# Attention and two feed-forward stages on one core: normalising ahead of the next maximum, and the q copy on ScalarE

## The chip, the cores and the metric

One core of a Trainium2 chip. The time is the device time of the whole kernel in microseconds; of a kernel's runs the median counts.

## What is computed

Windowed and pooled attention over q, k, v of shape (2, 8, 576, 64), then a routed mixture of 8 experts, then a feed-forward layer. The change lies in the attention, of which this is the core:

```python
factor = 4
q_d = q.reshape(B, H, Sd, factor, D).mean(axis=3)        # k_d, v_d alike
out_d = sm_attn(q_d, k_d, v_d)                           # softmax attention, pooled
out_up = np.repeat(out_d, factor, axis=2)
mask = np.abs(pos[:, None] - pos[None, :]) < factor
scores = scale * np.matmul(q, k.transpose(0, 1, 3, 2))   # scale = 1/8
scores = np.where(mask, scores, -1000000000.0)
scores = scores - np.max(scores, axis=-1, keepdims=True)
attn = np.exp(scores)
attn = attn / (np.sum(attn, axis=-1, keepdims=True) + 1e-09)
out_local = np.matmul(attn, v)
return (out_up + out_local).astype(np.float32)
```

Its result, as 1152 tokens of 512 numbers, is routed to one expert each (`w1`, ReLU, `w2`, times the gate), and the outcome goes through `x @ w_in`, `h * tanh(softplus(h))`, `@ w_out`.

## The kernel before

Each engine has its own program, a block of instructions in a fixed order, and they meet at semaphores. The attention handles the 1152 tokens in 9 tiles of 128. Its work is cut into 15 steps, written out in the list `STEPS`: 9 local steps (one tile each, all 8 heads, a window of 70 keys for each 64 queries) and 6 pooled steps ("down") in the order local 0 to 3, three down, three down, local 4 to 8. A loop `for n in range(ROUNDS)`, with 19 rounds, runs on every engine and spreads each step over several rounds.

TensorE in round n: some warming matmuls on constant data (`keep_warm`, rounds 0 to 9), `scores(n)`, the transposes of k and then q of tile n + 2 (rounds 0 to 6, `transpose_k`, L1116; `transpose_q`, L1108), from round 9 on the transposes and logits for the router, `attend` of an earlier step, and `probs_t(n - 1)`, the transposes of the probabilities (L1173 for a local step, L1168 for a pooled one). `probs_t` of a local step waits for `s_nrm`, that is for `norm` of its step on VectorE; that of a pooled step waits for the exponentials alone, as its factor is applied later, in `od_copy`. It also waits for `s_ptc`, the copy of the transposed probabilities before it. `scores(n)` waits for the exponentials of step n - 2 and for the copies of q and k; round 4 and round 7, the first pooled steps of each batch, also for the pooled sums (`s_qd`). In rounds 10 to 14 the counts of the router stand in the middle of `scores(n)` and wait for VectorE's one-hot sums (`s_cum`, L938).

VectorE in round n: `stats(n)` (the negated row maximum of the scores, from PSUM, L881 or L877 and L879; in rounds 10 to 14 behind `read_counts`), `q_copy(n + 2)` (q times 1/8 from PSUM into `qT`, L854), `norm(n - 1)` (L888, sum plus a small number; L890, its reciprocal; L893, in local steps, probabilities times the reciprocal), the router's `place`, `pooled` sums of q and k over 4 tokens (L840; tile 0 in round 0, tile 1 in round 1, tiles 2 and 3 in round 2, tile 4 in round 3, and so on to tiles 7 and 8 in round 6), `od_copy` and `route`.

ScalarE in round n: the router's copies and exponential, `k_copy(n + 2)` (L646), `exps(n)` (8 exponentials of 70 columns or 4 of 144, L663, each with its row sum), `pt_copy(n - 1)` (the transposed probabilities out of PSUM, L646) and `x_copy` (the attention's output, L646). `exps(n)` waits for the maximum of its step (`s_mx`).

GpSimd builds constant rows, adds up v for the pooled steps (`sum_v`, L545 to L548), places pooled outputs and scatters rows of x to the experts. SyncE's queue issues the loads in a fixed order: q and k of tiles 0 to 5, v for the pooled steps, tiles 6 to 8 (from tile 3 on a load waits until the tile three before it has been transposed), more v, the router's weights, 22 loads of windows of v (L422), zeros for the experts' rows, and then the experts' weights.

Of the kernel before, what the change touches and what calls it, by code (L numbers as in the profile page):

```python
# [7 lines left out]
P = 128  # L8
# [6 lines left out]
ALU = mybir.AluOpType  # L15
# [118 lines left out]
def build(nc, q, k, v, w_gate, w1, w2, w_in, w_out, consts, consts16, out, cap):  # L134
# [12 lines left out]
    with ctx:  # L147
# [134 lines left out]
        def turned(n):  # L282

            return n + 2 if 0 <= n < NT - 2 else None
# [356 lines left out]
        def _(act):  # L641
# [3 lines left out]
            def copy(dst, src):  # L645
                return nc.scalar.activation(dst, src, ACT.Copy)  # L646

            def k_copy(t):
                act.wait_ge(s_tk, t + 1)
                copy(kT[:, :, HALO + t * P:HALO + (t + 1) * P],  # L650
                     ps[:, qk_banks(t)[1], :].rearrange("p (h t) -> p h t", h=HP)).then_inc(s_kTc, 1)
# [47 lines left out]

            for t in range(2):  # L700
                k_copy(t)
            act.wait_ge(s_cb, 5)
            for n in range(ROUNDS):
                if x_turn(n) is not None:
                    xt_copy(x_turn(n))
                if count_turn(n) is not None and n < ROUNDS - 1:
                    gate_exp(count_turn(n))
                if turned(n) is not None:
                    k_copy(turned(n))
                if n < NS:  # L710
                    exps(n)
                if is_local(n - 2) and n - 2 in attended(n):
                    x_copy(n - 2)
                if 0 <= n - 1 < NS:
                    pt_copy(n - 1)
                for m in attended(n):
                    if is_local(m) and m != n - 2:
                        x_copy(m)
# [102 lines left out]
        def _(dve):  # L821
# [27 lines left out]
                    last = red(kdT[:, :, kcol:kcol + cnt], kT[:, :, HALO + lo:HALO + lo + n])  # L849
                last.then_inc(s_qd, 1)  # L850

            def q_copy(t):
                dve.wait_ge(s_tq, t + 1)
                V.tensor_scalar(qT[:, :, t * P:(t + 1) * P], ps[:, q_bank(t), :].rearrange("p (h t) -> p h t", h=HP),  # L854
                                SCALE, None, ALU.mult).then_inc(s_qTc, 1)

            def views(n):

                s0 = 2 * (n % 2)
# [105 lines left out]
                need(gate)  # L965
                V.tensor_scalar(x_sb[:, t, :], x_sb[:, t, :], r_gate[:, c], None, ALU.mult).then_inc(s_gx, 1)

            for t in range(2):
                q_copy(t)
            for n in range(ROUNDS):  # L970
                if n < NS:
                    stats(n, count_turn(n))
                if turned(n) is not None:
                    q_copy(turned(n))
                if 0 <= n - 1 < NS:
                    norm(n - 1)
                if count_turn(n) is not None:
                    if n >= NS:
                        read_counts(count_turn(n))
# [470 lines left out]
```

## Time and profile before

| | |
|---|---|
| median of 3 runs | 483.32 us (481.43 to 490.93) |
| profiled execution, as timed | 488.61 us |
| its span, first to last instruction | 486.5 us |
| mean granted clock of TensorE | 0.966 |
| TensorE matmul busy | 454.6 us, 93% of the span |
| VectorE busy | 275.3 us, 57% |
| ScalarE busy | 229.3 us, 47% |
| GpSimd busy | 134.9 us, 28% |

A row of the timeline gives a start and a duration in us from the span's start, the engine (PE is TensorE, DVE VectorE, ACT ScalarE, POOL GpSimd, SPq SyncE's queue), the line, the operation, and what it writes and reads; the last brackets are the idle time in front of it and who ended it. A granted clock of 1.00 is 2.4 GHz, 0.50 is 1.2 GHz. An instruction's duration has a fixed tail that overlaps with the next one's start, so that the distance between two starts is what one costs in a row of its like.

### The profile page before, as it was taken

Reading aid. Unit: us, or ns where it says so; the run is one execution under the profiler, and the core shown is the slowest. Engines: PE = TensorE matmul, PEld = TensorE weight load, DVE = VectorE, ACT = ScalarE, POOL = GpSimd, SP = SyncE. Lnnn points to the kernel's source line nnn. Section 1 sums busy time; section 2 is a strip of 40 time slices with the busy share of each in tenths; the row PEclk is TensorE's granted clock in tenths of the full one; section 3 lists DMA queues with packets and bytes.
Section 4 is the critical chain, followed back from the end, with each engine's and each line's share of the span. In section 5 each row is a group of like instructions: output and inputs, shape, how many; then the busy total and the mean of one; then the engine's idle time right before and its main releaser. Section 6 shows DMA issues by size and latency. Waiting matters only on the chain.

```text
span 486.5 us, 10257 instructions
## 1 busy us (share of the span) xinstructions
PE 454.6 (93%) x3520; PEld 420.3 (86%) x3521; DVE 275.3 (57%) x660; ACT 229.3 (47%) x629; POOL 134.9 (28%) x133
## 2 busy tenths in 40 slices
PE   9756899988879999999999999999999999999993
PEld 8645798778779999999999988899999888899982
DVE  5575647878211111011111399888888888888883
ACT  2653467860312333233224366665655565765541
POOL 8484332412000000000000565433352223443202
PEclk9876999997989999999999999999999999999998
DMA  9969898412558799897775314231232121141001
GB/s 186 190 117 170 156 369 287 154 66 101 194 173 293 265 348 328 276 328 268 269 243 188 121 44 83 48 87 44 88 108 86 43 80 50 54 142 43 1 0 65
DMA packets 72001, 74.87 MB, mean 154 GB/s; under 512 B 32800, under 2 KB 47776, under 8 KB 71968
## 3 DMA queue, kind: packets, MB, share of 16 engines
q1 hardware_dynamic: 70240, 69.71, 48.4%
q0 software_dynamic: 1728, 4.72, 2.5%
q8 instruction: 20, 0.33, 0.3%
q14 instruction: 13, 0.11, 0.1%
HBM read 64.98 MB, written 9.44 MB: 153 GB/s over the span
## 4 chain that ended last, share of the span: by engine, by line
PE 85%; DVE 8%; issue 2%; ACT 2%; DMA 1%; POOL 0%; POOLq 0%; SPq 0%; ACTq 0%; DVEq 0%
PE ps L1097 79%; PE ps L1173 1%; PE ps L1312 1%; DVE pr L893 1%; PE ps L1116 1%; PE ps L1168 1%; PE ps L1108 1%; DVE qT L854 1%; DMA xg<-x_by_expert 1%; DMA x_by_expert<-x_sb,xslot 1%; DVE sme L888 1%; PE ps L1218 0%; ACT pr L663 0%; ACT prT L646 0%; DVE kdT L840 0%
## 5 line engine op out<-in xcount | busy, mean ns | idle before, releaser
L597 POOL TENSOR_TENSOR wiL<-raw,wiH 128x512 fp32r<-128x512 f32 x48 | 62.4, 1302 | 259.5 <-ACT wiH L646 156.1
L1097 PE MATMUL ps<-hid,raw 128*128 128x128 f32 (+2 forms) x512 | 72.3, 301 | 3.4 <-issue 3.4
L1097 PEld LDWEIGHTS ps<-hid,raw 128*128 128x128 f32 x512 | 70.4, 195 | 3.6 <-issue 3.6
L1097 PE MATMUL ps<-xe,raw 128*128 128x128 f32 (+2 forms) x512 | 70.3, 298 | 1.4 <-issue 0.8
L1097 PEld LDWEIGHTS ps<-xe,raw 128*128 128x128 f32 x512 | 68.8, 191 | 2.3 <-issue 1.4
L1097 PE MATMUL ps<-x2L,wiH 128*128 128x384 f32 x192 | 65.3, 340 | 0.0
L1097 PE MATMUL ps<-x2H,wiH 128*128 128x384 f32 x192 | 65.1, 339 | 0.2 <-DVE x2L L1013 0.2
L1097 PE MATMUL ps<-x2H,wiL 128*128 128x384 f32 x192 | 64.6, 337 | 0.0
L1097 PE MATMUL ps<-woH,gH 128*128 (+1 forms) x144 | 56.9, 395 | 1.9 <-DVE gL L1013 1.9
L1097 PE MATMUL ps<-woH,gL 128*128 (+1 forms) x144 | 57.1, 397 | 0.0
L1097 PE MATMUL ps<-woL,gH 128*128 (+1 forms) x144 | 56.7, 394 | 0.0
L1013 DVE TENSOR_TENSOR woL<-wo_in,woH 128x1024 f32 x8 | 9.8, 1226 | 81.2 <-ACT woH L646 81.2
L785 ACT ACTIVATE md<-mg 128x384 f32<-128x384 f32 x48 | 25.3, 526 | 43.3 <-DVE mg L1068 43.2
L741 ACT ACTIVATE hid<-ps 128x128 f32<-128x128 f32 (+2 forms) x64 | 18.6, 301 | 51.5 <-PE ps L1097 47.2
L1050 DVE TENSOR_SCALAR mu<-ps 128x384 f32<-128x384 f32 x48 | 26.7, 557 | 25.3 <-PE ps L1097 25.3
L1097 PEld LDWEIGHTS ps<-x2H,wiH 128*128 128x128 f32 x192 | 36.0, 188 | 2.4 <-issue 0.5
L1013 DVE TENSOR_TENSOR x2L<-ps,x2H 128x128 f32 (+2 forms) x32 | 9.3, 321 | 50.8 <-ACT x2H L646 50.7
L1097 PEld LDWEIGHTS ps<-x2L,wiH 128*128 128x128 f32 x192 | 36.1, 188 | 1.9
L646 ACT ACTIVATE gH<-ps 128x384 fp32r<-128x384 f32 x48 | 23.6, 492 | 26.9 <-DVE ps L1074 26.9
L1097 PE MATMUL ps<-warmb 128*128 128x160 bf16 x320 | 33.1, 277 | 3.3 <-DVE kdT L840 1.8
L1097 PEld LDWEIGHTS ps<-x2H,wiL 128*128 128x128 f32 x192 | 36.0, 188 | 0.0
L1097 PEld LDWEIGHTS ps<-warmb 128*128 128x128 bf16 x320 | 30.8, 119 | 4.1 <-issue 3.0
(130 smaller groups left out, 770.7 us busy)
## 6 DMA issues: line engine op xcount, KB each, us to landing
raw<-in_moe_w SPq DMA_DIRECT2D x32, 1024.0 KB, 6.4
raw<-in_moe_w_in SPq DMA_DIRECT2D x24, 512.0 KB, 3.7
x_by_expert<-x_sb SPq DMA_DIRECT2D x1, 4608.0 KB, 15.8
xg<-x_by_expert SPq DMA_DIRECT2D x8, 512.0 KB, 3.7
wo_in<-in_moe_w_out SPq DMA_DIRECT2D x8, 512.0 KB, 7.4
v<-in_v SPq DMA_DIRECT2D x4, 576.0 KB
qk_tok<-in_k SPq DMA_DIRECT2D x8, 256.0 KB, 4.4
qk_tok<-in_q SPq DMA_DIRECT2D x8, 256.0 KB, 5.0
```

The costliest lines, as they stand in the source:

```text
L597: nc.gpsimd.tensor_tensor(wiL[:, r, :, :], raw_wi_tile(r), wiH[:, r, :, :].bitcast(F32), ALU.subtract).then_inc(s_wil, 1)
L646: return nc.scalar.activation(dst, src, ACT.Copy)
L741: nc.scalar.activation(hid[:, m, 0:w], ps[:, m % 4, 0:w], ACT.Relu).then_inc(s_hr, 1)
L785: nc.scalar.activation(d, mg[:, r1, :], ACT.Ln, bias=2.0).then_inc(s_ln, 1)
L854: V.tensor_scalar(qT[:, :, t * P:(t + 1) * P], ps[:, q_bank(t), :].rearrange("p (h t) -> p h t", h=HP), SCALE, None, ALU.mult).then_inc(s_ ...
L888: V.tensor_scalar(st(sme), st(sm), f, f * EPS, ALU.mult, ALU.add).then_inc(s_den, 1)
L893: V.tensor_tensor(pb, pb, st(rc).unsqueeze(3).to_broadcast(shape), ALU.mult).then_inc(s_nrm, 1)
L1013: V.tensor_tensor(dst, whole, high.bitcast(F32), ALU.subtract).then_inc(sem_, 1)
L1050: V.tensor_scalar(mu[:, r, :], ps[:, 3 + r, 0:SW], MISH_CAP, None, ALU.min).then_inc(s_uc, 1)
L1097: return T.matmul(out_, a, b, start=start, stop=stop, skip_group_check=True)
L1108: last = T.transpose(ps[:, q_bank(t), hp * P:(hp + 1) * P], qk_tok[:, slot3, 0, hp * P:(hp + 1) * P], ident)
L1116: last = T.transpose(ps[:, qk_banks(t)[1], hp * P:(hp + 1) * P], qk_tok[:, slot3, 1, hp * P:(hp + 1) * P], ident)
```

## The change

VectorE's `q_copy` goes to ScalarE, where it stands behind `k_copy` of the same tile and in front of `exps`, as an activation Copy with scale 1/8; the first two are made ahead of the loop, as before. On VectorE, `norm(n - 1)` moves to the head of the round, in front of `stats(n)`.

```diff
--- before.py
+++ after.py
@@ -645,6 +645,11 @@
             def copy(dst, src):
                 return nc.scalar.activation(dst, src, ACT.Copy)
 
+            def q_copy(t):
+                act.wait_ge(s_tq, t + 1)
+                nc.scalar.activation(qT[:, :, t * P:(t + 1) * P], ps[:, q_bank(t), :].rearrange("p (h t) -> p h t", h=HP),
+                                     ACT.Copy, scale=SCALE).then_inc(s_qTc, 1)
+
             def k_copy(t):
                 act.wait_ge(s_tk, t + 1)
                 copy(kT[:, :, HALO + t * P:HALO + (t + 1) * P],
@@ -699,6 +704,7 @@
 
             for t in range(2):
                 k_copy(t)
+                q_copy(t)
             act.wait_ge(s_cb, 5)
             for n in range(ROUNDS):
                 if x_turn(n) is not None:
@@ -707,6 +713,7 @@
                     gate_exp(count_turn(n))
                 if turned(n) is not None:
                     k_copy(turned(n))
+                    q_copy(turned(n))
                 if n < NS:
                     exps(n)
                 if is_local(n - 2) and n - 2 in attended(n):
@@ -849,11 +856,6 @@
                     last = red(kdT[:, :, kcol:kcol + cnt], kT[:, :, HALO + lo:HALO + lo + n])
                 last.then_inc(s_qd, 1)
 
-            def q_copy(t):
-                dve.wait_ge(s_tq, t + 1)
-                V.tensor_scalar(qT[:, :, t * P:(t + 1) * P], ps[:, q_bank(t), :].rearrange("p (h t) -> p h t", h=HP),
-                                SCALE, None, ALU.mult).then_inc(s_qTc, 1)
-
             def views(n):
 
                 s0 = 2 * (n % 2)
@@ -965,15 +967,11 @@
                 need(gate)
                 V.tensor_scalar(x_sb[:, t, :], x_sb[:, t, :], r_gate[:, c], None, ALU.mult).then_inc(s_gx, 1)
 
-            for t in range(2):
-                q_copy(t)
             for n in range(ROUNDS):
+                if 0 <= n - 1 < NS:
+                    norm(n - 1)
                 if n < NS:
                     stats(n, count_turn(n))
-                if turned(n) is not None:
-                    q_copy(turned(n))
-                if 0 <= n - 1 < NS:
-                    norm(n - 1)
                 if count_turn(n) is not None:
                     if n >= NS:
                         read_counts(count_turn(n))
```

## Rows read from the trace of the kernel before

**Rows 1.** The page's 40 slices of the span: TensorE's busy tenths, its granted clock.

```profile
PE   9756899988879999999999999999999999999993
...
PEclk9876999997989999999999999999999999999998
```

**Rows 2.** Windows by stage: busy us (instructions) of each engine, granted clock, DMA share, GB/s.

```profile
12.50:60.00 47.50, 34.17 (x361) 28.96 (x358) 30.14 (x56) 23.73 (x101) 23.96 (x26) 0.78 0.85 157
60.00:75.00 15.00, 15.00 (x263) 13.18 (x262) 6.21 (x22) 8.79 (x30) 6.87 (x13) 1.00 1.03 350
```

**Rows 3.** Waits of TensorE, 11 to 60 us: waited for, us in all, times, longest.

```profile
PE ps L1173 <- DVE pr L893: 11.1, 4, 3.7
```

**Rows 4.** Timeline of TensorE: start us, us, instruction, [idle before, ended by].

```profile
13.95 0.99 PE L1097 MATMUL ps<-warmb 128*128 128x160 bf16 x12 [0.41 <-ACT kT L646]
...
15.76 0.66 PE L1116 MATMUL ps<-cst,qk_tok 128*128 128x128 f32 x4
...
18.87 1.08 PE L1173 MATMUL ps<-cst,pr 128*70 128x128 f32 x8 [2.02 <-DVE pr L893]
19.75 1.80 PE L1097 MATMUL ps<-warmb 128*128 128x160 bf16 x12
...
27.54 1.92 PE L1173 MATMUL ps<-cst,pr 128*70 128x128 f32 x8 [3.34 <-DVE pr L893]
...
45.41 1.92 PE L1173 MATMUL ps<-cst,pr 128*70 128x128 f32 x8 [3.74 <-DVE pr L893]
...
51.49 0.82 PE L1168 MATMUL ps<-cst,pr 96*72 96x96 f32 x8
...
58.76 1.27 PE L1097 MATMUL ps<-warmb 128*128 128x160 bf16 x16 [1.66 <-DVE kdT L840]
...
105.24 1.04 PE L1173 MATMUL ps<-cst,pr 128*70 128x128 f32 x8
```

**Rows 5.** Timeline of VectorE, rounds 1, 2 and 4.

```profile
15.90 0.74 DVE L881 TENSOR_REDUCE mx<-ps 128x8 f32<-128x560 f32 x1 [0.44 <-PE ps L1097]
16.89 0.69 DVE L854 TENSOR_SCALAR qT<-ps 128x512 f32<-128x512 f32 x1 [0.25 <-PE ps L1108]
17.50 0.16 DVE L888 TENSOR_SCALAR sme<-sm 128x8 f32<-128x8 f32 x1
...
17.93 0.80 DVE L893 TENSOR_TENSOR pr<-pr,rc 128x560 f32<-128x560 f32 x1
...
24.84 0.85 DVE L888 TENSOR_SCALAR sme<-sm 128x8 f32<-128x8 f32 x1
...
25.96 1.52 DVE L893 TENSOR_TENSOR pr<-pr,rc 128x560 f32<-128x560 f32 x1
...
42.32 1.25 DVE L888 TENSOR_SCALAR sme<-sm 128x8 f32<-128x8 f32 x1
```

**Rows 6.** Timeline of ScalarE: the first and the last of round 1's exponentials.

```profile
16.95 0.31 ACT L663 ACTIVATE pr<-ps,mx 128x70 f32<-128x70 f32 x1
...
19.21 0.25 ACT L663 ACTIVATION_READ_ACCUMULATOR pr<-ps,mx 128x1 f32 x1
```

**Rows 7.** A window after the first stall, columns as in rows 2.

```profile
19.75:23.10 3.35, 3.35 (x49) 2.76 (x46) 0.17 (x1) 1.02 (x1) 0.57 (x2) 0.50 0.95 202
```

**Rows 8.** ScalarE's k copies as a group: busy us, mean ns, idle before.

```profile
L646 ACT ACTIVATE kT<-ps 128x512 f32<-128x512 f32 x9 | 5.4, 602 | 22.6 <-PE ps L1116 22.6
```

**Rows 9.** Timeline of GpSimd: copies, then the first and last of six sums.

```profile
15.28 5.04 POOL L564 COPY raw<-cst 32x512 f32<-32x512 f32 x8 [3.94 <-DMA cst<-in_consts]
24.40 1.26 POOL L545 TENSOR_TENSOR vd<-v 72x512 f32<-72x512 f32 x1 [4.08 <-DMA v<-in_v]
...
31.33 1.26 POOL L548 TENSOR_TENSOR vd<-vd,v4s 72x512 f32<-72x512 f32 x1
```

**Rows 10.** Waits of TensorE, 75 to 116 us, columns as in rows 3.

```profile
PE ps L1097 <- DVE cum L938: 2.6, 5, 0.8
```

**Rows 11.** Timeline of the queue of loads (SyncE): the windows of v.

```profile
37.45 22.27 SPq L422 DMA_DIRECT2D vwin<-in_v  x22
```

## Prediction

> **What bounds the kernel now.** I read the page's slices first [rows 1]: TensorE is busy in nine tenths or more of most slices, and the clock that it is granted is down to 0.6 to 0.8 in the second to fourth slice, that is from 12 to 49 us. The windows by stage say the same in microseconds [rows 2]: from 12.5 to 60 us TensorE works 34.17 of 47.5 us at a mean clock of 0.78, from 60 to 75 us 15.00 of 15.00 at 1.00. From the twelfth slice on nearly all is TensorE's own work, and the change doesn't touch it. So I look at the first 60 us, and a little at 75 to 116 us.
>
> Who ends TensorE's idle time there is in the waits [rows 3]: four times, 11.1 us in all, the transposes of the probabilities (L1173, `probs_t`) wait for the multiplication on VectorE (L893, in `norm`). One more wait, 1.66 us in front of 58.76 [rows 4], is for the pooled sums of k (L840). The timeline of TensorE [rows 4] gives the order of one round: warming matmuls and scores (from 13.95), transposes of k and q of the tile after next (15.76), then `probs_t` of the round before (18.87), 2.02 us late. VectorE's rows [rows 5] say why: it takes the maximum (15.90), then waits for the q transposes to copy q (16.89), and only then normalises (17.50 to 18.73). ScalarE [rows 6] is ready long before: the exponentials of round 1 run from 16.95 to 19.46 and are normalised at 24.84, in round 2. So the stall is an order on VectorE: `norm(n-1)`, ready long before, stands behind `stats(n)` and `q_copy(n+2)`, which need TensorE's newest work. `probs_t` of rounds 0 to 3 should come one TensorE round apart; it starts at 18.87 and, three rounds later, at 45.41 [rows 4], 8.85 us apart.
>
> Each of these stalls is followed by matmuls at the lower clock [rows 7]: 19.75 to 23.10 at 0.50 (1.2 GHz), after an idle 2.02 us. Twelve warming matmuls take 1.80 us there and 0.99 us at 13.95 at the higher level (2.4 GHz) [rows 4]; sixteen took 1.27 us at 58.76, so that after 1.66 us of idleness the clock was still the higher one.
>
> **The change part by part.**
>
> *q copy to ScalarE.* Nine copies leave VectorE, 0.69 us each [rows 5]; ScalarE copies k from the same kind of PSUM bank in 602 ns [rows 8], 0.5 us from start to start. I take 0.5 us of ScalarE for each q copy, between 0.5 (a k copy's pitch) and 0.69 (VectorE's time), 4.5 to 6.2 us in all. ScalarE sat idle 22.6 us in front of the k copies alone, so it has room; but the copy stands in front of `exps(n)`, so it delays them by 0.5 to 0.7 us where the maximum is there already. In the first two copies, ahead of the loop, 26 warming matmuls cover it: nothing.
>
> *norm ahead of the maximum.* The new chain goes in a circle: `exps(n)` 2.5 us (16.95 to 19.46 [rows 6]), `norm(n)` 1.23 us, `stats(n+1)` 0.75 us [rows 5], with hand-overs of 0.05 to 0.1 us: 4.6 us a round. TensorE's round at full clock is 1.81 for warming and scores (13.95 to 15.76), 0.93 for the transposes (0.49 and 0.44, the k transposes' pitch and the q's) and 0.88 for `probs_t` (18.87 to 19.75), 3.6 us [rows 4]; at the lower one 3.35 (19.75 to 23.10 [rows 7]) and, doubled, 1.7 and 1.7: 6.8 us. What waits behind `norm` on VectorE is the maximum, behind it ScalarE's exponentials, and behind these the copy of the transposed probabilities: nothing that TensorE needs in the same round.
>
> How long `norm` takes depends on GpSimd. At 17.50 to 18.73 it took 1.23 us; at 24.84 to 27.48 it took 2.64 us (the small L888 0.85 instead of 0.16, L893 1.52 instead of 0.80 [rows 5]), and GpSimd's first sums of v, six in a row, run from 24.40 to 32.6 [rows 9]. In round 4 the small one alone took 1.25 (42.32), about 3.0 in all. The same instructions in the same place would give both prices again, so I use 2.64 inside 24.4 to 32.6 us and 1.23 outside.
>
> The Trainium skill, "GPSIMD Engine Reference", section Key points, says that GpSimd shares its SBUF interfaces with VectorE and contends with instructions that have two SBUF inputs, which L893 is. By that rule alone the normalisation at 17.93, under GpSimd's copies (15.28 to 20.3 [rows 9]), would be slow too; the row has 0.80 us there, so only the sums are charged. Were every one of the four charged, the sum would be 2.8 us smaller.
>
> *The walk.* Round 0: the k copy ends just before 13.95, where TensorE was waiting for it; the q copy behind it lets `exps(0)` start at about 14.2 and end at 16.7. Round 1: `norm(0)` 16.75 to 18.0, `probs_t(0)` at 18.1 (was 18.87); maximum to 18.75, `exps(1)` 18.8 to 21.3. Round 2: TensorE's transposes end at 18.1 + 0.88 + 1.81 + 0.93, with their tail 21.9; `norm(1)` runs 21.3 to 22.65, before the sums of v begin; `probs_t(1)` at 22.75 (was 27.54). Maximum to 23.35, `exps(2)` to 25.9. Round 3: TensorE is through at 26.6, `norm(2)` is charged 2.64: `probs_t(2)` at 28.6, idle 2.0 us. Maximum to 29.25, pooled sums of tile 4 to 30.6, and the warming matmuls of round 4 start there. `exps(3)` to 31.8, `norm(3)` partly charged: `probs_t(3)` at 34.0 (was 45.41): 11.4 us early. Round 5 at full clock is 0.88 + 1.1 + 0.66 + 0.93 = 3.6 us, so `probs_t(4)` is at 37.7 (was 51.49); from there to the end of `probs_t(5)` it is 5.6 us (51.49 to 58.76 less 1.66 [rows 4]): 43.3. The 1.66 us wait for pooled sums behind it shrinks to about 0.3, since VectorE no longer has the q copy in front. Warming matmuls of round 7 at 43.6 instead of 58.76: 15.2 us.
>
> One stall of the walk, 2.0 us, is as long as the ones after which the clock fell. A fall would put some 4 us of TensorE's work at half speed, half of it inside waits: 2 us back. I take that: 13.2 us.
>
> *Rounds 7 to 11* have next to no idle TensorE (15.00 of 15.00 us from 60 to 75 [rows 2]) and don't change: `norm` first finds `exps` done and fills the time in which VectorE waits for the scores. *Rounds 12 to 14*: VectorE's one-hot sums hold the counts up for 2.6 us in five waits [rows 10]. `norm` now runs while VectorE waits for the scores, so the sums come earlier, until TensorE's own round is the limit. Three of the five waits lie where no scores are left and stay. Between 0 (the sums hang on the logits anyway) and 1.0 us (two, of 0.52 us on average); I take 0.9.
>
> *Moved transfers.* The queue of loads issues 22 loads of v in 22.27 us from 37.45 on [rows 11]; a load ahead of them waits for the transposes of tile 5, which the walk brings from about 34 (27.54 + 1.7 + 3.35 + 1.3) to 26.5. With the loads between, they start some 5 us earlier, at 32.5; eleven of them, one batch, are issued by 43.6, and the first use is in round 8, after 51 us. That covers the landing; nothing is charged. If they did not move at all, 2 to 3 us would be lost.
>
> Sum: 13.2 + 0.9 = 14.1 us from the profiled execution, 486.5 us of span and 488.61 us as timed: 474.5. The median before, 483.32, is 5.3 us below that execution. If none of this difference lies in the first 60 us, the median goes to 469.2. If part of it is a clock that fell less often, that part can't be won: a mean clock of 0.78 is 0.44 of 47.5 us at half speed, 21 us, of which up to 13 can be idle, so the clock cost between 4 and 10 us there. I discount 14.1 to 11.8 and predict 471.5 us.
>
> **The rivals.**
>
> *The clock stays low.* With every round at 6.8 us TensorE itself is the limit: `probs_t(3)` at 18.1 + 3 x 6.8 = 38.5, 6.9 us early, plus 1.3 and 0.9: 9.1 us from the profiled execution. Discounted like the forecast, 475.5 (473.5 to 479). For: the walk leaves stalls of 1.3 and 2.0 us. Against: 1.66 us did no harm. The same time comes out if the executions of the kernel before that make the median had a high clock: then its rounds take 3.6 + 0.7 (q copy) + 1.23 or 2.64 (`norm`) + 0.15, 5.7 to 7.1 us, against 4.6 to 5.9, so about 5 + 1.3 + 0.9 = 7 us in all. Together 0.25.
>
> *Transfers become the bound*: qk tiles or v blocks land late. The mean DMA share is 0.85 in 12.5 to 60 us [rows 2], and TensorE has no wait for a load among its waits. Against that, the shift asks for the same bytes sooner. 4 to 8 us back of the 11.8: 475.5 to 479.5. Chance 0.12.
>
> *The circle is the new bound and gives nothing.* From `probs_t(0)` to `probs_t(14)` the rounds average 6.2 us now (18.87 to 105.24 [rows 4]). If exponentials, normalisation and maximum take 6.2 us in each, nothing is won: about 483. That needs `norm` charged everywhere and slow hand-overs. Chance 0.08.
>
> *Slower.* The same circle in all 14 rounds at 6.9 us or more gives 0.7 x 14 = 10 us: 493. It decides where `norm` passes 3.5 us; the longest in rows 5 is about 3.0, in one round. Chance 0.04.
>
> **How the numbers follow.** Forecast 0.51, with its own range of 466 to 474.5. About 2% (9.7 us, below 473.7) is what a measurement can tell. Faster takes most of the forecast's share and some of the first two rivals': 0.57. Slower: 0.04. Same: 0.39. The range 466 to 479.5 leaves out the last two rivals and thin tails.
>
> **What would show it.** Right: the waits of TensorE for L893's successor fall from 11.1 us to under 5; `probs_t` of round 3 starts near 34; the granted clock between 20 and 50 us is above 0.9; the gap in front of round 7's warming matmuls is under 1 us; the expert phase starts 12 to 15 us earlier. Wrong: TensorE waits for the transposed probabilities' copy or for k and q to land; the clock in 20 to 50 us is still near 0.7; ScalarE's exponentials wait for the maximum for more than 1 us in rounds 7 to 14.

## The result and the profile after

| | before | after |
|---|---|---|
| median of the first comparison | 484.50 us (481.43 to 490.93, 4 executions) | 478.50 us (477.59 to 479.58, 4) |
| ratio after/before, 95% interval | | 0.9881, 0.9833 to 0.9929 |
| profiled execution, as timed | 488.61 us | 479.58 us |
| span | 486.5 us | 477.5 us |
| mean granted clock of TensorE | 0.966 | 0.982 |

The kernel became 1.2% faster. It was timed twice more, with the same sign: 476.64 us (ratio 0.9879) and 478.09 us (0.9832). The medians here are of all executions, while the ratios leave out slow ones, more than 1.5% above the fastest of the same kernel. The forecast was 471.5 us: the time lies in the range of 466 to 479.5 us, but the gain came out at half to four fifths of what was forecast. It was 6.0, 9.5 and 8.0 us by the medians of the three comparisons and about 6, 6 and 8 us by the ratios, instead of 11.8.

The slices of the span on the profile's page, TensorE's busy tenths and its granted clock, which answer [rows 1]:

```profile
PE   9778999878699999999999999999999999999993
...
PEclk9979899999999999999999999999999999999998
```

The windows by stage (columns as in [rows 2]), with a window of 5.2 us behind the longest stall:

```profile
12.50:60.00 47.50, 39.73 (x532) 34.79 (x522) 30.11 (x61) 32.12 (x127) 28.61 (x34) 0.89 0.98 166
60.00:75.00 15.00, 15.00 (x262) 13.37 (x261) 11.16 (x49) 10.09 (x44) 4.04 (x8) 1.00 1.04 377
...
31.30:36.50 5.20, 5.17 (x32) 4.61 (x33) 3.41 (x7) 2.60 (x10) 4.51 (x6) 0.50 1.00 207
```

TensorE is busy for 39.73 of the first 47.5 us instead of 34.17, at a clock of 0.89 instead of 0.78. Its waits from 11 to 60 us, against [rows 3]:

```profile
PE ps L1171 <- DVE pr L895: 4.5, 3, 2.5
PE ps L1095 <- DVE kdT L847: 2.8, 2, 1.8
```

The waits for the normalised probabilities fell from 11.1 to 4.5 us. The waits for the pooled sums of k grew from 1.8 us in all (0.16 and 1.66) to 2.8 us (0.98 and 1.84). TensorE's timeline, with the rows that answer [rows 4]:

```profile
18.61 1.04 PE L1171 MATMUL ps<-cst,pr 128*70 128x128 f32 x8 [1.45 <-DVE pr L895]
19.48 0.99 PE L1095 MATMUL ps<-warmb 128*128 128x160 bf16 x12
...
22.94 1.07 PE L1171 MATMUL ps<-cst,pr 128*70 128x128 f32 x8 [0.55 <-DVE pr L895]
...
29.28 1.07 PE L1171 MATMUL ps<-cst,pr 128*70 128x128 f32 x8 [2.53 <-DVE pr L895]
31.33 2.29 PE L1095 MATMUL ps<-warmb 128*128 128x160 bf16 x16 [0.98 <-DVE kdT L847]
...
36.52 1.49 PE L1171 MATMUL ps<-cst,pr 128*70 128x128 f32 x8
...
48.08 2.29 PE L1095 MATMUL ps<-warmb 128*128 128x160 bf16 x16 [1.84 <-DVE kdT L847]
```

`probs_t` of rounds 0 to 3 starts at 18.61, 22.94, 29.28 and 36.52 instead of 18.87, 27.54, 36.04 and 45.41. Sixteen warming matmuls take 2.29 us at 31.33 and at 48.08, against 1.27 us at 58.76 in [rows 4]: the clock fell twice, once behind idle times of 2.53 and 0.98 us with only `probs_t`, still at the higher clock, between them, and once behind 1.84 us. VectorE, against [rows 5] (the multiplication of rounds 0 and 1, then round 2):

```profile
17.61 0.85 DVE L895 TENSOR_TENSOR pr<-pr,rc 128x560 f32<-128x560 f32 x1
...
22.14 0.74 DVE L895 TENSOR_TENSOR pr<-pr,rc 128x560 f32<-128x560 f32 x1
...
26.12 1.19 DVE L890 TENSOR_SCALAR sme<-sm 128x8 f32<-128x8 f32 x1 [0.21 <-ACT pr L668]
...
27.59 1.64 DVE L895 TENSOR_TENSOR pr<-pr,rc 128x560 f32<-128x560 f32 x1
```

The normalisation of round 2 lies under GpSimd's sums and lasts from 26.12 to about 29.2, 3.1 us. ScalarE's copies as groups (against [rows 8]) and the loads of v (against [rows 11]):

```profile
L646 ACT ACTIVATE kT<-ps 128x512 f32<-128x512 f32 x9 | 5.5, 611 | 12.8 <-PE ps L1114 12.8
L650 ACT ACTIVATE qT<-ps 128x512 f32<-128x512 f32 x9 | 5.4, 605 | 0.3 <-PE ps L1106 0.3
```

```profile
34.86 22.68 SPq L422 DMA_DIRECT2D vwin<-in_v  x22
```

A q copy costs ScalarE 605 ns, 0.5 us from start to start. The loads moved by 2.6 us, from 37.45 to 34.86, and TensorE still waits for none of them.

### The profile page after: what moved, and what is told of

It reads as the page before. It is cut to its first block, busy times and chain, and to the rows that moved or that the text cites. A ratio compares the mean times of both kernels' runs of the same rounds, so it can differ in the third digit from the quotient of the medians.

```text
span 477.5 us, 10260 instructions
## 1 busy us (share of the span) xinstructions
PE 449.0 (94%) x3520; PEld 415.5 (87%) x3521; DVE 271.6 (57%) x651; ACT 233.6 (49%) x638; POOL 134.9 (28%) x133
## 4 chain that ended last, share of the span: by engine, by line
PE 83%; DVE 6%; ACT 5%; issue 3%; DMA 1%; POOL 0%; another core or an unknown queue 0%; POOLq 0%; SPq 0%; DVEq 0%; ACTq 0%
PE ps L1095 78%; ACT pr L668 3%; PE ps L1310 1%; DMA xg<-x_by_expert 1%; PE ps L1166 1%; PE ps L1114 1%; PE ps L1171 1%; DVE mx L883 1%; ACT prT L646 1%; DMA x_by_expert<-x_sb,xslot 1%; DVE sme L890 1%; PE ps L1216 0%; POOL out L618 0%; DVE kdT L847 0%; DVE gL L1011 0%
## 5 line engine op out<-in xcount | busy, mean ns | idle before, releaser
L1095 PE MATMUL ps<-hid,raw 128*128 128x128 f32 (+2 forms) x512 | 70.9, 297 | 3.6 <-issue 3.6
L1095 PEld LDWEIGHTS ps<-hid,raw 128*128 128x128 f32 x512 | 69.0, 191 | 3.8 <-issue 3.8
L668 ACT ACTIVATE pr<-ps,mx 128x70 f32<-128x70 f32 (+2 forms) x96 | 30.6, 343 | 10.5 <-DVE mx L881 7.0
L1095 PE MATMUL ps<-warmb 128*128 128x160 bf16 x320 | 30.7, 265 | 4.3 <-DVE kdT L847 2.8
```

What stands on the lines that cost most here:

```text
L668: last = nc.scalar.activation(pr[0:rows, n % 2, a, h * w:(h + 1) * w], ps[0:rows, 2 * (n % 2) + a, h * w:(h + 1) * w], ACT.Exp, bias=mx[0: ...
L1095: return T.matmul(out_, a, b, start=start, stop=stop, skip_group_check=True)
```

## The experiments

First the kernels against themselves. The profile of each shows how far one execution speaks for the kernel.

> The kernel before, unchanged, for a second trace of it and for what the comparison itself scatters. Both theories: ratio 1.00 within 0.5%. Theory A (the order on VectorE): the four waits for L893 come out near 11 us again. Theory B (the clock): where an execution of this kernel is shorter than the one in rows 1 to 11, its granted clock from 12.5 to 60 us is above 0.78 and its first warming matmuls of round 7 start before 58.76 us.

> The kernel after, unchanged, in the same call as its two halves. Expected ratio 0.980 to 0.990, span near 477 us, waits of TensorE for L895 near 4.5 us from 11 to 60 us. If the stop of all engines near 80 us in the first trace (TensorE 0.35 us, VectorE 2.1 us, ScalarE 2.75 us idle until 80.1 to 80.2) belongs to the kernel, it is there again within 2 us of that place; if it is chance, it is not.

> The kernel after once more, as the reference of this call. Expected: 476.5 to 479, ratio of the medians of all runs to before 0.980 to 0.985.

Measured: `b0_again` 486.6 us (ratio 1.0034, 0.9984 to 1.0084), `a0_again` 476.64 us (0.9879, 0.9813 to 0.9944), `a0_third` 478.09 us (0.9832, 0.9785 to 0.9880). In the profile of `b0_again` the four waits for L893 come to 9.8 us, not quite the 11 expected, and the execution was a longer one, 491.08 us; it comes up again below. An execution of the kernel after whose clock was 0.96 from 12.5 to 60 us (`a0_again`, TensorE's timeline):

```profile
28.31 1.07 PE L1171 MATMUL ps<-cst,pr 128*70 128x128 f32 x8 [2.08 <-DVE pr L895]
30.35 1.27 PE L1095 MATMUL ps<-warmb 128*128 128x160 bf16 x16 [0.98 <-DVE kdT L847]
...
34.02 1.07 PE L1171 MATMUL ps<-cst,pr 128*70 128x128 f32 x8 [0.71 <-DVE pr L895]
...
45.28 2.29 PE L1095 MATMUL ps<-warmb 128*128 128x160 bf16 x16 [1.96 <-DVE kdT L847]
```

Here 2.08 and 0.98 us of idleness left the clock at its higher level, and `probs_t` of round 3 stands at 34.02, where the walk had 34.0. The 1.96 us ahead of round 7 did let it fall.

### Which of the two edits does it

`e1_norm_first` moves `norm` alone; the q copy stays on VectorE:

```diff
             for n in range(ROUNDS):
+                if 0 <= n - 1 < NS:
+                    norm(n - 1)
                 if n < NS:
                     stats(n, count_turn(n))
                 if turned(n) is not None:
                     q_copy(turned(n))
-                if 0 <= n - 1 < NS:
-                    norm(n - 1)
```

> The first half alone: norm ahead of stats on VectorE, the q copy stays on VectorE behind stats. Theory A (only the order matters): TensorE's waits for L893 fall to about 5 us as in the kernel after, ratio 0.985 to 0.990; the q copy costs VectorE 0.6 us a round in a circle that does not hold it, but delays pooled sums by 0.6 us in rounds 3 and 6, so 1 us slower than the kernel after. Rival (both halves needed): with the q copy still between the maximum and the pooled sums the waits only halve, and the ratio is 0.993 or more.

`e2_q_on_act` moves the q copy alone; from the kernel after, `norm(n - 1)` goes back behind `stats(n, ...)`.

> The second half alone: q copies on ScalarE, norm still behind stats. Theory A: norm(n-1) no longer waits for the q transposes (0.93 us) nor for the copy (0.6 us), but still for the scores and the maximum: it ends about 1.2 us earlier a round, waits for L893 6 to 7 us instead of 11.1, 4 to 5 us gained plus what the clock gives back; ratio 0.988 to 0.993. Rival (norm first carries everything): under 1 us gained, ratio 0.998 to 1.00.

Measured: 478.59 us, ratio 0.9865 (0.9792 to 0.9937), and 477.52 us, 0.9886 (0.9830 to 0.9942); `a0_again`, in the same comparison, 0.9879. Each edit alone gives what both give together, as far as intervals of 0.6 to 0.7% either way can tell. TensorE's waits for the normalised probabilities are 4.1 us with `norm` moved alone (about 5 expected) and 5.8 us with the q copy moved alone (6 to 7 expected). `probs_t` of rounds 0 to 3 starts at 18.17, 22.88, 28.55 and 34.08 with the q copy moved alone. They are two ways to the same end: the stall was there because `norm` stood behind a copy that needs TensorE's newest transposes. With the copy gone, only the maximum is left in front, whose scores are ready before those transposes.

### Does `norm` on the pooled rounds hurt?

In `e7_norm_first_local_only` `norm(n - 1)` stands first only where step n - 1 is local, and behind `stats` where it is pooled:

```diff
-                if 0 <= n - 1 < NS:
+                if is_local(n - 1):
                     norm(n - 1)
                 if n < NS:
                     stats(n, count_turn(n))
+                if is_down(n - 1):
+                    norm(n - 1)
```

> The kernel after, with norm ahead of the maximum only for local steps; for pooled steps, whose norm is two small instructions that TensorE doesn't wait for, it stands behind stats again. Theory (in rounds 5 to 7 norm first delays maximum and pooled sums): in round 6 the maximum starts when the scores end, about 1.0 us earlier, the wait for L847 in front of round 7 falls from 1.9 to about 1 us and the clock stays up behind it: 474 to 476, 1 to 2.5 us under the kernel after. Rival (the pooled sums are bound by the last copies): no change within 0.5 us.

Measured: 479.99 us, 0.9870 (0.9799 to 0.9940). The wait in front of round 7 shrank from 1.84 and 1.96 to 0.93 us, and the clock held there: round 7 at 43.84, the walk's 43.6. So that wait does come from `norm(5)`, which waits for its exponentials and holds back the maximum and the pooled sums behind it. But at 54.97 TensorE then waited 2.87 us for GpSimd's copies of the pooled outputs (L556), the clock fell there, and nothing was left: the first count came at 64.65, against 62.3 to 65.7 us in the profiles of after, and the time is no better.

### The price of GpSimd's sums, and of the clock

`e3_sums_later` keeps GpSimd's sums of v out of the first four normalisations:

```diff
             pool.wait_ge(s_rep, 2 * HELD)
+            pool.wait_ge(s_nrm, 4)
             for j in range(KH):
```

> The kernel after, with GpSimd's sums of v held back until the fourth local normalisation is done. Theory (GpSimd's sums slow norm, and the long stall in round 3 is theirs): norm(2) takes 1.2 us instead of 3.1, TensorE's wait in round 3 falls from 2.1 to 2.5 us to about 0.8, probs_t(3) starts 1.5 to 2.5 us earlier, at 32 to 33; the sums then fall on the rounds of pooled steps and slow VectorE's small instructions there, so of these 2 us about 1 is left: 475.5 to 477, ratio 0.976 to 0.990. Rival (norm is slow for another reason): norm(2) still takes over 2.5 us and the time is that of the kernel after.

`e4_warm_first` puts the warming matmuls ahead of the waits for q and k, so that they fill TensorE's idle time:

```diff
+                    if n == FIRST_DOWN[1]:
+                        pe.wait_ge(s_qTc, NT)
+                    if is_down(n) or STEPS[n][1] < HELD:
+                        keep_warm(2 * (n % 2), WARM_DOWN if is_down(n) else WARM_LOCAL)
                     if n in FIRST_DOWN:
...
-                    if is_down(n) or STEPS[n][1] < HELD:
-                        keep_warm(2 * (n % 2), WARM_DOWN if is_down(n) else WARM_LOCAL)
```

> The kernel after, with the warming matmuls of a round in front of its waits for q, k and the pooled sums (in round 7 behind the wait for the last q copy alone) instead of behind them. Theory (what is left in rounds 4 and 7 is a wait and the clock that it lets fall): the 2.9 us of waits for L847 shrink to about 0.9, since 1.2 us of warming run inside each, and the clock in round 7 stays at 1.00, which gives 1.5 us more: 472.5 to 475, 3 us under the kernel after. Rival (the wait sets the round whatever runs in front of it): the scores of round 7 start no earlier than now, under 1 us gained.

`e6_before_stalls_warm` fills the stalls of the kernel before with warming matmuls, ahead of `probs_t` in rounds 1 to 4:

```diff
+                if 1 <= n <= HELD:
+                    pe.wait_ge(s_exp, n)
+                    keep_warm(2 * ((n + 1) % 2), 24)
```

> The kernel before, with 24 more warming matmuls (2 us at the higher clock) in rounds 1 to 4 between the transposes and probs_t, where TensorE waits 1.9 to 3.7 us for norm. They take no time from the chain, as VectorE ends later. Theory (half of the stalls' price is the clock after them): granted clock from 12.5 to 60 us rises from 0.78 to 0.83 to over 0.93, the time falls from 486 to 479 to 481 us though every wait for norm is still there in its end, and the scatter between executions falls from 11 us to about 5. Rival (the stalls themselves are the price): waits plus warming stay at 11 us and the time within 2 us of 486.

Measured: e3 480.91 us, 0.9906 (0.9841 to 0.9971); e4 482.34 us, 0.9941 (0.9873 to 1.0009); e6 487.01 us, 1.0008 (0.9933 to 1.0084). Windows of e4 and of e6:

```profile
12.50:60.00 47.50, 40.07 (x602) 35.07 (x603) 33.24 (x73) 35.16 (x138) 30.92 (x38) 1.00 0.96 173
```

```profile
12.50:60.00 47.50, 42.02 (x589) 37.36 (x587) 33.30 (x66) 28.59 (x119) 28.07 (x33) 0.96 0.94 180
```

In e3 the small L891 takes 0.17 us in rounds 2 and 3 again instead of 1.19 and 0.65, and `probs_t` comes at 26.68 and 31.52; but the sums then fall upon the pooled rounds, the clock fell at 43.18, and the first experts' transposes start at 114.8, as in the profile of after. The slow normalisation is GpSimd's work, and moving it gains nothing. In e4 the clock stays at 1.00 and round 7 starts at 42.67, 5.4 us earlier than in the profile of after, yet the time looks worse than that of the kernel after, by 3 to 5 us by the ratios and 4 to 6 us by the medians. The intervals of the ratios overlap, and the kernel after did not run in that comparison, so that only this is sure: nothing of the 3 us that were expected was gained. The counts end at 103.1, and the part behind the first experts' transposes takes 367.7 us instead of 362.7 to 364.9. In e6 the profiled execution has its counts at 106.45, 8 us earlier than in the profile of the kernel before (114.38), and took 482.73 us; the other three took 486.4 to 488.4 us. The 479 to 481 us expected if the clock behind the stalls were half their price did not come. Filling the stalls, without removing them, is worth nothing that was measured.

`f3_after_no_warm` and `f4_before_no_warm` take the warming matmuls of rounds 0 to 9 out of the kernel after and of the kernel before:

```diff
-WARM_LOADS, WARM_TILE, WARM_DOWN, WARM_LOCAL, WARM_COUNTS, WARM_SCATTER = 50, 14, 16, 12, 8, 90
+WARM_LOADS, WARM_TILE, WARM_DOWN, WARM_LOCAL, WARM_COUNTS, WARM_SCATTER = 50, 14, 0, 0, 8, 90
```

> The kernel after without the warming matmuls of rounds 0 to 9; nothing that is computed changes. Theory A (in the kernel after TensorE no longer waits, and the warming matmuls keep the clock up): without them TensorE idles more than 1 us in each of rounds 0 to 6, the granted clock from 12.5 to 60 us is 0.7 or below, and the counts end at 104 us or later: 478 to 484 us. Theory B (the round is set by the circle of exponentials, normalisation and maximum, and the warming only fills it): the counts end at 98 to 102 us, and the time is 473 to 477 us.

> The kernel before without the warming matmuls of rounds 0 to 9. Theory A (the change wins by taking stalls away, each of which costs a fall of the clock): with no warming the clock is low in both kernels' first 60 us, the stalls are still there in this one, and it is slower than the kernel before, 486 to 495 us, with a distance to the kernel after without warming of 7 us or more. Theory B (the clock alone is what the two kernels differ by): the distance to the kernel after without warming is under 4 us.

Measured: 480.48 us, 0.9881 (0.9823 to 0.9940), and 485.23 us, 0.9966 (0.9919 to 1.0012). The clock of 12.5 to 60 us is 0.75 and 0.78, alike, and the kernels still stand 4.8 us apart, with the counts 5.4 us apart (102.96 and 108.41); by the ratios they are some 4 us apart. That lies at or above the 4 us of one expectation and below the 7 us of the other: most of what the change is worth, 6 to 8 us, doesn't need the clock. The warming itself gives the kernel before nothing, though 486 us or more was expected without it; the kernel after without warming lies between its two expectations, at 480.48 us with the counts' end at 102.96; for the kernel after the ratios leave it open (0.9881 is also what it had in the first comparison, 0.9832 in the last).

### Where executions of the kernel before differ

> The kernel before once more, for a third profile. If what the executions of the kernel before differ by is the granted clock in the first 60 us, an execution with a clock of 0.85 or more there has its round 7 at 55 us or earlier and takes under 485 us, and one at 0.78 takes 487 to 491 us. If they differ in the expert phase, round 7 is at 55 to 59 us whatever the time.

> The kernel before, one more profile. Theory A (executions of the kernel before differ by how often the clock falls behind the stalls of rounds 1 to 4): an execution with a mean clock of 0.975 or more shows 0.87 or more in 12.5 to 60 us, round 7 at 55 us or earlier, and takes under 485 us; one at 0.964 to 0.968 shows 0.78 to 0.84 there, round 7 at 57 to 59 us, and takes 487.5 to 491 us. Theory B (they differ in the expert phase): round 7 stays at 55 to 59 us at either time, and the clock differs behind 105 us.

Measured: `b0_look` 489.65 us at a mean clock of 0.964, `b0_look2` 482.53 us at 0.979. Windows of 12.5 to 60 us, first `b0_look`, then `b0_look2`:

```profile
12.50:60.00 47.50, 34.06 (x376) 29.11 (x375) 30.66 (x57) 23.68 (x101) 24.89 (x27) 0.82 0.86 158
```

```profile
12.50:60.00 47.50, 35.49 (x477) 30.67 (x469) 31.73 (x65) 26.35 (x111) 26.92 (x30) 0.93 0.87 160
```

TensorE's timeline in `b0_look2`:

```profile
19.62 1.11 PE L1173 MATMUL ps<-cst,pr 128*70 128x128 f32 x8 [2.42 <-DVE pr L893]
20.53 1.81 PE L1097 MATMUL ps<-warmb 128*128 128x160 bf16 x12
...
27.55 1.92 PE L1173 MATMUL ps<-cst,pr 128*70 128x128 f32 x8 [2.58 <-DVE pr L893]
...
35.05 1.07 PE L1173 MATMUL ps<-cst,pr 128*70 128x128 f32 x8 [2.19 <-DVE pr L893]
36.45 1.27 PE L1097 MATMUL ps<-warmb 128*128 128x160 bf16 x16 [0.33 <-DVE kdT L840]
...
41.28 1.07 PE L1173 MATMUL ps<-cst,pr 128*70 128x128 f32 x8 [1.87 <-DVE pr L893]
42.18 1.27 PE L1097 MATMUL ps<-warmb 128*128 128x160 bf16 x16
...
52.78 1.27 PE L1097 MATMUL ps<-warmb 128*128 128x160 bf16 x16 [2.20 <-DVE kdT L840]
```

It is the same program with the same four stalls. Behind 2.42 us the clock fell (1.81 us for twelve warming matmuls); behind 2.19, 1.87 and 2.20 us it did not (1.27 us for sixteen). Round 7 starts at 52.78 instead of 57.61 and the counts end at 108.43 instead of 113.60: 5.2 of the 7.1 us between the two executions lie there. Both came out as the first theory of each expectation has it.

`b0_again` shows that the first 60 us are not all. Its clock from 12.5 to 60 us was 0.83 and its round 7 starts at 55.17, before the 58.76 of the first profile, and yet at 491.08 us it is the longest of all. Its fall came at round 7:

```profile
55.17 2.29 PE L1097 MATMUL ps<-warmb 128*128 128x160 bf16 x16 [2.90 <-DVE kdT L840]
```

From 60 to 75 us its clock was 0.84, the counts end at 115.13, later than the 114.38 of the first profile, and the part behind them takes 373.9 us instead of 372.1.

The Trainium skill, "TensorE: Matmul & The Clock Gate", Part 1: The HAM clock gate, says that what it watches is free-running, so that the same kernel runs different numbers of matmuls at the low clock from run to run. The profiles agree with that, without showing the cause: 2.42 us of idleness let the clock fall and 2.20 us in the same execution did not, while 1.84 us did in the profile of after. The edges lie wider still. The clock fell directly behind 1.31 us at 46.92 in `e8_weights_held` (further down) and behind 1.42 us at 44.80 in e2, and held behind 2.53 us at 47.89 in e1.

Over all comparisons, 76 executions of the kernel before have a clock on record. They lie between 479.84 and 491.08 us, median 485.96, mean clock 0.976, and a line through them falls by 3.6 us for each 0.01 of mean clock (correlation -0.89). Of the 14 executions of the kernel after the median is 477.96 and the mean clock 0.981. Fitted together, the change is worth 6.0 us at equal clock (standard error 0.4), and the rest, about 2 us, goes with the clock: 0.005 times 350 to 360 us. The execution on which the forecast was built had 0.966; only 10 of the 76 have 0.967 or less.

`b9_before_more_warm` has 14 instead of 12 warming matmuls in a local round (`WARM_LOCAL = 14`).

> The kernel before with 14 instead of 12 warming matmuls in each local round (0 to 3, 7 to 9): 0.17 us more of TensorE's work in a round at full clock, 0.30 at half. Theory A (the clock of the first 60 us decides which of its executions is fast, and idleness of TensorE decides the clock): the waits shrink by the work that is added, a fall is somewhat rarer, the mean clock of its executions rises to 0.976 or more, and the median is 1 to 3 us lower, 482 to 485 us. Theory B (VectorE's order sets the rounds, the clock or not): the median is within 1 us of the kernel before.

Measured: 485.75 us (479.81 to 490.58), 0.9991 (0.9938 to 1.0043): no difference, and the same spread. A little more warming doesn't steady the clock.

### What is given back near 77 us

From round 7's warming to the end of the counts, the kernel before takes 55.6, 60.0, 56.0 and, in `b0_look2`, 55.7 us; the kernel after 57.7, 56.6 and 58.0, and e3, e7, e4 and e9, which are earliest at round 7, 62.8, 61.0, 60.4 and 63.2.

Part of this lies ahead of the counts. From round 7's warming to the first of them it is 16.2 to 16.5 us in the three profiles of before whose clock held at round 7, 17.6 to 17.8 us in all three of after, whose clock fell there, and 20.5 to 20.8 us in `b0_again`, e3 and e7. From the first to the last count it is 39.3 to 39.5 us in the profiles of before and 40.1, 38.9 and 40.2 us in those of after.

In two of three profiles of after, and in e3, e4, e7, e8 and e9, VectorE stops for 2.1 to 3.0 us between 72 and 82 us and ScalarE with it, for 1.2 to 2.8 us. TensorE's idle time there is shorter, 0.35 us in the profile of after. For VectorE's wait the trace names no releaser on the core. VectorE in the profile of after:

```profile
80.17 0.17 DVE L946 TENSOR_TENSOR prod<-ps,oh 128x8 f32<-128x8 f32 x1 [2.10 <-remote]
```

The third distance between two rounds of counts is 4.9 us in `a0_again`, e1 and f1 and 5.3 to 5.8 us in the other profiles without such a stop; it is 6.1 us here, and 7.2 to 7.7 us in e3, e4 and e9. So the stop costs about 1 us (0.3 to 1.2, by what it is set against), and some 2 us in those three. I had two suspects: the queues, which are full until then with the experts' weights, and GpSimd's first scatters in a row:

```profile
77.30 1.15 POOL L587 DMA_INDIRECT x_by_expert<-x_sb,xslot  x1 [0.29 <-POOL vwin L556]
78.76 0.96 POOL L587 DMA_INDIRECT x_by_expert<-x_sb,xslot  x1 [0.31 <-issue]
```

`e8_weights_held` holds the first expert's weights back until later steps are attended. `e9_warm_first_weights_held` is the same on e4, `b8_before_weights_held` on the kernel before:

```diff
             for i in range(4):
-                sp.wait_ge(s_av, RANK[local_step(i)] + 1)
+                sp.wait_ge(s_av, RANK[local_step(max(i, 5))] + 1)
                 load_unit(0, i)
```

> The kernel after, with the four loads of expert 0's weights (4 MB) held until local step 5 has been attended (round 13, about 84 us) instead of local steps 0 to 3 (from 58 us on). Theory (what was won by round 7 is partly given back because rounds 11 to 13 now run while the zeros' write and these loads fill the DMA engines, and code arrives late): DMA share between 75 and 85 us falls from 1.0 to under 0.6, no engine shows a stop of 1.5 us or more ended by nothing in the trace in rounds 11 to 13, and the time from round 7's warming matmuls to the last count falls from 56.6 to 62.8 us to 55.5 to 56: 474.5 to 476, about 2 us under the kernel after. Rival (chance, or the loads are then late for the experts): same time within 0.7 us, or 1 to 3 us slower with expert 0 waiting for its weights.

> Warming matmuls in front of the waits, and the weights' loads held as well. Theory: e4_warm_first was 2.7 us ahead at the warming of round 7 and lost it to stops near 77 us and in expert 0; with the loads held it keeps them: 472 to 475 and the last count before 101 us. Rival (the later stages cost this whatever the DMA engines do): over 479 as e4_warm_first.

> The kernel before with the same loads held (its round 13 is near 94 us). Its rounds 11 to 13 come at 82 to 98 us, when its DMA share is already 0.64 and falling, and its trace has no stop there, so theory: within 1 us of before, ratio 0.998 to 1.002. Rival (holding the loads is good or bad in itself): the same change of 2 us or more as in e8_weights_held.

Measured: 480.48 us, 0.9897 (0.9840 to 0.9955); 482.80 us, 0.9862 (0.9793 to 0.9932), a ratio that rests on two of four executions; 487.69 us, 1.0009 (0.9963 to 1.0055). None of the gains that were expected came. In e8 the DMA share of 70 to 85 us falls to 0.04 to 0.27, and the stop is there as before, 2.1 us. Full queues are not its cause.

`f1_scatter_held` lets the scatters start only when five tiles are multiplied by their gates:

```diff
             pool.wait_ge(s_zf, 16)
+            pool.wait_ge(s_gx, 5)
             for t in range(NT):
```

> The kernel after, with one wait more on GpSimd: its scatters of x start only when five tiles are multiplied by the gate, so that they come some rounds later than 77 us. Theory A (the stop of all engines by about 2 us near 74 to 80 us belongs to the first scatters in a row): the stop leaves that place, or moves with the scatters, and the counts' rounds near 78 us are 5.3 to 5.8 us long; the counts end at 101 to 104 us. Theory B (the stop belongs to the place in the work, or to a transfer of another queue): a stop of 1.7 to 3 us is still there between 72 and 82 us, with no scatter near it. In both the last scatters come no later than in the kernel after, since the order behind the fifth tile is the same: 475 to 480 us.

Measured: 479.60 us, 0.9848 (0.9783 to 0.9913). There is no stop between 72 and 82 us, and the third distance of the counts is 4.9 us. But among the scatters, which now come one behind the other from 90.33 on, ScalarE has a wait without a releaser on the core:

```profile
90.33 1.15 POOL L588 DMA_INDIRECT x_by_expert<-x_sb,xslot  x1 [14.43 <-DVE x_sb L969]
91.79 1.51 POOL L588 DMA_INDIRECT x_by_expert<-x_sb,xslot  x1 [0.30 <-issue]
...
97.06 1.02 ACT L647 ACTIVATE prT<-ps 70x1024 f32<-70x1024 f32 x1 [2.99 <-remote]
```

VectorE works on until 96.45 us, so that it is not the same stop. The counts, expected to end at 101 to 104 us, end at 107.5: the two distances between counts that fall among the scatters are 4.8 and 7.0 us, against 4.2 and 4.1 in the profile of after. What speaks for the scatters is that the stop left its place with them, and that time was lost where they went. What speaks against them as a full account is `a0_again`, where three scatters in a row (75.19, 76.65, 78.11) stopped nothing, as did none in the profiles of the kernel before (86.41 and 87.86 in `b0_look`). The mechanism stays open. Nor did it pay to hold the scatters: no variant was faster than the kernel after by more than the noise.

## Why the prediction was wrong

**The mechanism was right.** The stall was an order on VectorE, `norm` behind the q copy, and it went. The waits fell under 5 us (4.5), `probs_t` of round 3 came at 34.02 and 33.34 in two profiles of three (36.52 in the first), and the loads of v were hidden (they moved by 2.6 us, not by 5). q copies at 0.5 us a piece and the rounds' length held: 4.3, 5.9 and 5.7 us from one `probs_t` to the next in `a0_again`, where the walk had 4.65, 5.85 and 5.4. Three signs of being right failed. The clock of 20 to 50 us was 0.85 in the first profile, below the 0.9 that I wanted (0.94 in the two others). The gap in front of round 7 was 1.84 to 1.96 us, not under 1. The experts' first transposes came 8.3 us earlier in the first pair of profiles and 11.1 us on the mean of three (112.1 us against 123.2), not 12 to 15. One sign of being wrong appeared and told nothing: in rounds 7 to 14 the exponentials wait for the maximum twice, 6.5 us in all and 4.9 us at the longest, but in the kernel before it was 5.5 us, and 3.8 us at the longest.

**Two steps failed**, the sum and the way from the profiled execution to the median. The miss is 6.5 us, 478.0 (the median of the 14 executions of the kernel after, and the mean of its three profiled ones) against 471.5.

**The sum: 3.5 us.** It took the profiled execution from 488.61 down to 474.5 us; the kernel after takes 478.0. Its own three profiles show where, on their mean:

| | the sum | kernel after | late by |
|---|---|---|---|
| warming of round 7 starts | 45.6 us | 46.0 us | 0.4 us |
| from there to the first count | 16.35 us, as before | 17.7 us | 1.3 us |
| from the first count to the last | 39.3 us, as before, less 0.9 | 39.8 us | 1.4 us |
| behind the last count | 372.1 us, as before | 372.5 us | 0.4 us |

Up to round 7 the walk was right on the mean, its 2 us for a fall of the clock included: 43.6 + 2 = 45.6. The term that failed there is the wait ahead of round 7, put at 0.3 us, which took 1.84 to 1.96. I let the q copy go from in front of the pooled sums, but not `norm(5)` come, which waits for its exponentials (L890 at 42.97 in the profile of after, 0.97 us long under GpSimd's second group of sums). Behind this wait the clock fell in all three profiles, where it had held behind 1.66 us in the profile of before. That is the 1.3 us of the second line, in rounds that the prediction took as unchanged. (Without it the 2 us would have been too much: in the two later profiles the clock held up to round 7, and the longer wait used them up.) The 0.9 us at the counts did not come, and where VectorE and ScalarE stop near 77 us, in two of the three profiles, about 1 us more went; the cause of that stop is open.

**The median: 3.0 us.** The median of three before, 483.32 us, lay 5.3 us below the profiled execution. The prediction saw the question ("if part of it is a clock that fell less often, that part can't be won") but took only 2.3 us off the gain, and so let the kernel after be 3.0 us faster than its own sum. The runs show no such 3.0 us: the profiled executions of the kernel after and its median agree, at 478.0. Of the 7.1 us between `b0_look` and `b0_look2`, 4.8 lie ahead of round 7, where the change takes the stalls away: against `b0_look2`, round 7 of the kernel after is only 6.8 us earlier (46.0 on average against 52.8) and the counts 5.0 us (103.4 against 108.4). And part of the 5.3 us was the luck of three executions: 483.32 us is 2.6 us below the median of the 76, 485.96, from which the profiled execution is only 2.7 us away. Against that median the gain is 8.0 us: the 10.7 that the sum should have given (488.61 less 477.96), less 2.7. In this light the discount of 2.3 us was about right by luck; the sum and the median of three carry the miss.

**The rivals.** What happened is nearest to the second half of the first rival, to which I gave 0.25 with its twin: executions of the kernel before with a high clock have shorter rounds, and about 7 us are won. `b0_look2` has rounds of 7.5 and 6.2 us behind its one fall, where that rival said 5.7 to 7.1. No transfer became the bound, and the circle of exponentials, normalisation and maximum had room: 4.3 to 5.9 us a round. The Trainium skill, "GPSIMD Engine Reference", section Key points, says that GpSimd contends with VectorE's instructions that read two SBUF inputs or run in a 2-port performance mode. The trace agrees for L895, with two inputs, under the sums (1.64 us instead of 0.74). L890, which reads one, was slowed more, from 0.17 to 1.19 us; in which mode it ran no row shows, so that the trace can't tell whether the rule covers it.

## What to carry to other kernels

A sum made on one profile gives the time of the kernel after; before it is put against a median, ask for each us between that profile and the median whether the kernel after would have it too, and take the median from more than three executions when they spread over 10 us. A stall's price includes the fall of the clock behind it, and that part is won only in the executions that paid it. A wait that grows can bring its own fall, and the price then lies in the stage behind it, here one that the prediction called unchanged. Two edits that shorten the same wait are not added: undo each alone. When a stage that feeds a loop is brought forward, look up for each instruction moved ahead what *it* waits for, in the rounds of every kind.

## What the runs showed of the hardware

- One program on one core ranged from 480 to 491 us, by 3.6 us for each 0.01 of the mean granted clock, with nothing else changed.
- The clock fell directly behind idle times of 1.31 (e8), 1.42 (e2), 1.84, 1.96 and 2.42 us and held behind 1.87, 2.08, 2.19, 2.20 and 2.53 us (e1). The length of a stall alone doesn't decide it.
- Under GpSimd's additions a VectorE instruction on 128x8 numbers took 0.52 (`a0_third`) to 1.25 us instead of 0.17; with the additions held out of the way (e3), it took 0.17 again. In the same stretch of the profile of after VectorE's reductions of 128x512 numbers were not slowed: 0.67 us at 24.64 and 25.24, under the additions, and 0.68 us at 23.46 and 24.05, ahead of them.
- Stops of VectorE (2.1 to 3.0 us, no releaser on the core) and ScalarE, with TensorE idle for less, came in 7 of 20 profiles and never in the kernel before. They stayed when the queues were emptied and were gone from their place when the scatters were held back.
